# First MLP, first product: tiles 6 to 17 in pairs by seven block products instead of eight

## The reference

```python
h = x @ w_in                                   # first MLP: 2304x512 by 512x1024
e = np.exp(h - h_max)
sm = e / (np.sum(e, axis=-1, keepdims=True) + 1e-09)
solu = h * sm
ln = (solu - mu) / np.sqrt(var + 1e-06) * g_ln
x = ln @ w_out                                 # 1024x512
...
h = x @ w_in2                                  # second MLP: 512x2048
g = np.maximum(h, 0.0) + np.log1p(np.exp(-np.abs(h)))
out = g @ w_out2                               # 2048x512
```

## Time and profile before

| | us |
|---|---|
| median of 3 runs | 874.36 (874.33 to 874.37) |
| the profiled execution, its own time | 873.95 |
| its span, first to last instruction | 872.2 |
| first MLP's steady part, three tiles | 36.0 |
| TensorE busy | 859.9 (99% of the span) |
| VectorE, ScalarE, GpSimd busy | 633.8, 566.5, 345.2 |

### The profile page before, as it was taken

One profiled execution on the slowest core, in us unless ns is written; L12 is line 12 of the kernel. 1 busy time (PEld: TensorE's weight loads), 2 busy tenths in 40 slices (PEclk: granted clock), 3 DMA queues, 4 the chain that ended last, 5 costly groups with the idle time before them and its releaser, 6 DMA issues.

```text
span 872.2 us, 17032 instructions
## 1 busy us (share of the span) xinstructions
PE 859.9 (99%) x6357; PEld 721.1 (83%) x6357; DVE 633.8 (73%) x1215; ACT 566.5 (65%) x1040; POOL 345.2 (40%) x498
## 2 busy tenths in 40 slices
PE   7999999999999999999999999999999999999998
PEld 5666666666677989889899999999999999999997
DVE  7999999999937361543656778758768768858975
ACT  4888988888876352533464766667667666667664
POOL 4676888676626310201111322333323322333331
PEclk9999999999999999999999999999999999999999
DMA  6813441343002000000032300000100100000000
GB/s 170 221 49 83 90 111 34 85 104 126 2 2 61 13 1 1 1 1 1 1 97 83 136 1 20 18 0 2 37 1 2 37 1 1 36 0 0 36 0 36
DMA packets 30234, 37.03 MB, mean 42 GB/s; under 512 B 4688, under 2 KB 18384, under 8 KB 30160
## 3 DMA queue, kind: packets, MB, share of 16 engines
q1 hardware_dynamic: 29776, 35.89, 14.9%
q10 hardware_dynamic: 384, 0.16, 0.1%
HBM read 31.33 MB, written 4.72 MB: 41 GB/s over the span
## 4 chain that ended last, share of the span: by engine, by line
PE 90%; DVE 5%; issue 2%; ACT 1%; POOL 1%; DMA 0%; SPq 0%; DVEq 0%; ACTq 0%
PE m_ps L1181 23%; PE f_ps L1274 23%; PE h_ps L1065 12%; PE y_ps L1205 12%; PE s_ps L1097 8%; PE o_ps L1138 7%; DVE ntop L870 3%; PE t_ps L1113 2%; DVE kept L880 1%; PE lt_ps L1217 1%; PE s_ps L1092 1%; ACT expd L606 1%; POOL thresh L470 1%; POOL w_lo L454 1%; PE l_ps L1108 0%
## 5 line engine op out<-in xcount | busy, mean ns | idle before, releaser
L1181 PE MATMUL m_ps<-y_hi,w 128*128 128x384 f32 x768 | 211.8, 337 | 0.0
L546 POOL TENSOR_TENSOR w_lo<-w_rest,w_hi 128x512 fp32r<-128x512 f32 x82 | 107.1, 1306 | 247.3 <-ACT w_hi L729 247.3
L1181 PEld LDWEIGHTS m_ps<-y_hi,w 128*128 128x128 f32 x768 | 140.3, 188 | 3.9
L606 ACT ACTIVATE expd<-s_ps,ntop 128x576 f32<-128x576 f32 x144 | 105.7, 742 | 40.4 <-DVE ntop L870 39.4
L1181 PE MATMUL m_ps<-y_lo,w 128*128 128x384 f32 x384 | 129.0, 336 | 0.0
L729 ACT CAST w_hi<-w_rest 128x512 fp32r<-128x512 f32 x82 | 51.0, 622 | 107.2 <-PE f_ps L1274 102.8
L880 DVE SCALAR_TENSOR_TENSOR kept<-s_ps,thresh,expd 128x576 f32<-128x576 f32 x144 | 112.4, 817 | 3.7 <-POOL thresh L470 0.6
L870 DVE TENSOR_REDUCE ntop<-s_ps 128x1 f32<-128x576 f32 x144 | 106.8, 757 | 8.7 <-PE s_ps L1097 2.7
L1274 PE MATMUL f_ps<-w_hi,g_lo 128*128 128x512 f32 x282 | 111.5, 395 | 0.0
L1274 PE MATMUL f_ps<-w_hi,g_hi 128*128 128x512 f32 x282 | 110.8, 393 | 0.0
L1274 PE MATMUL f_ps<-w_lo,g_hi 128*128 128x512 f32 x282 | 110.4, 392 | 0.0
(11 more groups left out here) (96 smaller groups left out, 1695.2 us busy)
## 6 DMA issues: line engine op xcount, KB each, us to landing
q_sb<-q_t SPq DMA_DIRECT2D x28, 288.0 KB, 5.0
v_sb<-v_main SPq DMA_DIRECT2D x16, 256.0 KB, 3.2
stage<-w_in SPq DMA_DIRECT2D x16, 256.0 KB, 2.8
out<-o_sb SPq DMA_DIRECT2D x5, 768.0 KB, 3.6
w_rest<-w_out SPq DMA_DIRECT2D x7, 512.0 KB, 5.4
k_sb<-k_t SPq DMA_DIRECT2D x21, 144.0 KB, 4.7
stage<-w_in SPq DMA_DIRECT2D x4, 512.0 KB, 7.9
stage<-w_out SPq DMA_DIRECT2D x4, 512.0 KB, 6.7
```

The lines of the kernel that those rows point to most:

```text
L546: nc.gpsimd.tensor_tensor(w4[1][n % 2], w4_rows(n % F2, 1)[:, 0, :], f32(w4[0][n % 2]), ALU.subtract).then_inc(w4lo_made, 1)
L606: nc.scalar.activation(expd[:, tile % 2, :].rearrange("p (a b) -> p a b", a=2), s_ps[tile % 2][:, :, 0:HALF], ACT.Exp, bias=ntop[:, tile % ...
L1181: last = nc.tensor.matmul(m_ps[n % 4][:, 0:GC], w[n % F2][:, k, :], y[odd][:, k, :], start=(k == 0 and m == 0), stop=(k == C - 1 and m == 2))
```

## The change

Tiles 0 to 5 (`PLAIN`) stay as they are. Tiles 6 to 17 are taken in six pairs, p = 3 to 8: tiles a = 2p and b = 2p + 1. For a pair the first product is one of 2x2 blocks: the two tiles by the two halves of the inner dimension on one side, the two halves of the inner dimension by the two sides of `w1` on the other. It is made from seven block products of 6 matmuls of 128x512 each (2 blocks x 3), 42 in place of 48. For that:

- `w1` is loaded again, 4 pieces of 512 KB, into the four slots of `stage`; the second MLP's pieces are loaded after these are used up. VectorE makes four differences T1 to T4 (128x1024 each, L1221), ScalarE casts them (L957), GpSimd subtracts for the low parts (L666).
- For each pair GpSimd makes four sums S1 to S4 of 128x256 (L647); ScalarE casts those and the three plain blocks (seven casts of 128x256, L944 to L951) and VectorE makes seven low parts (L1229 to L1239). The four operands x_hi, x_lo, x_sum have one slot each, so they are made when the pair before has been multiplied.
- The seven products go to the four banks of `h_ps`; ScalarE copies three out (128x512, L963), VectorE makes four sums of a bank and a copy (L1252), GpSimd three sums of 128x512 (L653 to L658). The result lies in `solu`, in SBUF, and the row chain reads it there.
- The transpositions stand inside the pairs (`transposed_in`): pairs 3, 5, 6 and 8 have three each, pairs 4 and 7 none. The projection follows in two or four chunks.

The core of the diff:

```diff
             for n in range(C):
+                sp.wait_ge(w_lo, parts(C + n + 1))
+                sp.dma_start(staged(n)[0], staged_source(n)).then_inc(stage_in[n], 16)
+            sp.wait_ge(wsum_made, 4)
+            for n in range(W3, W_ITEMS):
...
+            def joins(p):
+                pool.wait_ge(summed, first(p, SUMS, 2))
+                pool.wait_ge(copied, first(p, COPIES, 2))
+                nc.gpsimd.tensor_tensor(p5_sb, w_sb, p5_sb, ALU.add).then_inc(joined, 1)
+                pool.wait_ge(copied, first(p, COPIES, 3))
+                nc.gpsimd.tensor_tensor(w_sb, w_sb, p7_sb, ALU.add).then_inc(joined, 1)
+                pool.wait_ge(joined, first(p, JOINS, 1))
+                pool.wait_ge(ln_made, 2 * p)
+                nc.gpsimd.tensor_tensor(solu[:, 1, half(1)], p5_sb, p7_sb, ALU.add).then_inc(joined, 1)
+
+            def w1_sum_low(n):
+                pool.wait_ge(wsum_hi, n + 1)
+                pool.wait_ge(wsum_made, (2, 3, 4, 4)[n])
+                hi, lo = (T1, T2, T4, T3)[n]
+                raw = (T1_raw, T2_raw, T4_raw, T3_raw)[n]
+                nc.gpsimd.tensor_tensor(lo, raw, f32(hi), ALU.subtract).then_inc(wsum_lo, 1)
+
+            for tile in range(PLAIN - 1):
+                norm(0, tile)
+            x_sums_of(PAIRED[0])
+            norm(0, PLAIN - 1)
+            for n in range(4):
+                w1_sum_low(n)
+            for p in PAIRED:
+                joins(p)
+                if p + 1 in PAIRED:
+                    x_sums_of(p + 1)
+                for tile in (2 * p, 2 * p + 1):
+                    norm(tile // 6, tile % 6)
...
+            def paired(p):
+                tiles = transposed_in(p)
+                if tiles:
+                    next_row(tiles[0])
+                if p == PAIRED[0]:
+                    pe.wait_ge(solu_made, PLAIN)
+                else:
+                    pe.wait_ge(copied, first(p - 1, COPIES, 3))
+                    pe.wait_ge(summed, first(p - 1, SUMS, 4))
+                pe.wait_ge(xp_lo, first(p, OPERANDS, 1))
+                product(0, A11, B11)
+                pe.wait_ge(xp_lo, first(p, OPERANDS, 2))
+                product(1, A12, B21)
+                pe.wait_ge(xp_lo, first(p, OPERANDS, 4))
+                pe.wait_ge(wsum_lo, 1)
+                product(2, S1, T1)
+                if tiles:
+                    next_row(tiles[1])
+                pe.wait_ge(xp_lo, first(p, OPERANDS, 5))
+                pe.wait_ge(wsum_lo, 2)
+                product(3, S2, T2)
+                pe.wait_ge(copied, first(p, COPIES, 1))
+                pe.wait_ge(xp_lo, first(p, OPERANDS, 7))
+                pe.wait_ge(wsum_lo, 4)
+                product(0, S3, T3)
+                pe.wait_ge(summed, first(p, SUMS, 1))
+                pe.wait_ge(xp_lo, first(p, OPERANDS, 6))
+                product(1, S4, B22)
+                if tiles:
+                    next_row(tiles[2])
+                pe.wait_ge(copied, first(p, COPIES, 2))
+                pe.wait_ge(wsum_lo, 3)
+                product(2, A22, T4)
...
+            for p in PAIRED:
+                paired(p)
+                if p % 3 == 0:
+                    project(2 * (p // 3) - 1, (0, 1))
+                elif p % 3 == 1:
+                    project(2 * (p // 3) - 1, (2, 3))
+                else:
+                    if p == PAIRED[-1]:
+                        next_row(MT - 3)
+                    project(2 * (p // 3), range(C))
```

More of the change, by code:

```diff
@@ L61 @@
 W4_LOADS = 4
+PLAIN = 6
+PAIRED = range(PLAIN // 2, TOKENS // (2 * P))
+COPIES, SUMS, JOINS, PRODUCTS, OPERANDS, STEPS = 3, 4, 3, 7, 7, 6
+PADDED = 16
 GR = 4
@@ L792, in _, with at, x_pair_high @@
                     w_high(C + n - 2)
[L793 to L797, removed]
+            def at(tile):
+                return tile // 6, tile % 6
+            def x_pair_high(p, n):
+                a, b = 2 * p, 2 * p + 1
+                if n == 0:
+                    if p == PAIRED[0]:
+                        act.wait_ge(h_made, PLAIN)
+                    else:
+                        act.wait_ge(products, first(p, PRODUCTS, 0))
+                    for part, k in ((A11, 0), (A12, 2)):
+                        nc.scalar.copy(part[0], x_rows(a, k)).then_inc(xp_hi, 1)
+                elif n == 1:
+                    nc.scalar.copy(A22[0], x_rows(b, 2)).then_inc(xp_hi, 1)
+                else:
+                    act.wait_ge(xsum_made, first(p, 4, n - 1))
+                    raw = (S1_raw, S2_raw, S4_raw, S3_raw)[n - 2]
+                    nc.scalar.copy((S1, S2, S4, S3)[n - 2][0], raw).then_inc(xp_hi, 1)
@@ new lines, in y_copy @@
+            def y_copy(group, m):
+                act.wait_ge(y_made, C * group + m + 1)
+                nc.scalar.copy(xt[:, group * C * GC + m * GC:group * C * GC + (m + 1) * GC],
+                               y_ps[m % 2][:, 0:GC]).then_inc(y_out, 1)
+            row_exponential(0, 4)
+            transposed_high(0, 2)
+            row_square(0, 4)
+            x_pair_high(PAIRED[0], 0)
+            x_pair_high(PAIRED[0], 1)
+            row_exponential(0, 5)
+            w1_sum_high(0)
+            for n in range(2, STEPS):
+                x_pair_high(PAIRED[0], n)
@@ new lines, in at, with w1_sum @@
+            def at(tile):
+                return tile // 6, tile % 6
+            def w1_sum(n):
+                if n == 0:
+                    for slot in range(C):
+                        dve.wait_ge(stage_in[slot], 48)
+                    dve.wait_ge(h_made, PLAIN)
+                if n in (1, 2):
+                    dve.wait_ge(wsum_made, n)
+                r11, r12, r21, r22 = w1_again
+                out, x, y = ((T1_raw, r12, r11), (T2_raw, r22, T1_raw), (T4_raw, r21, T2_raw), (T3_raw, r22, r12))[n]
+                nc.vector.tensor_tensor(out, x, y, ALU.subtract).then_inc(wsum_made, 1)
@@ new lines, in _ @@
+            for s in range(2, PLAIN):
+                tile = s - 2
+                dve.wait_ge(h_made, tile + 1)
+                row_top(tile, h_ps)
+                x_low(0, s)
+                row_solu(tile, h_ps)
+                if tile >= 2:
+                    transposed_low(0, tile - 2)
+            dve.wait_ge(h_made, PLAIN - 1)
+            row_top(PLAIN - 2, h_ps)
+            row_solu(PLAIN - 2, h_ps)
+            transposed_low(0, 2)
+            dve.wait_ge(h_made, PLAIN)
+            row_top(PLAIN - 1, h_ps)
@@ L1256, in _, with next_row, product @@
-            three_parts(pe, MT + 3, 6, mlp1, MT // 6 - 1)
+            def next_row(tile):
+                pe.wait_ge(ltlo_made, tile)
+                transpose_row(tile)
+            def product(bank, x, w):
+                for k in range(2):
+                    for n, (part, other) in enumerate(((0, 0), (0, 1), (1, 0))):
+                        last = nc.tensor.matmul(banks[bank], x[part][:, k, :], w[other][:, k, :],
+                                                start=(k == 0 and n == 0), stop=(k == 1 and n == 2))
+                last.then_inc(products, 1)
```

337 lines of the change are left out of this document (260 added, 77 removed).

## The result

The changed kernel takes **876.91 us** (median of 9 runs, 874.84 to 877.57) against 874.37 (874.15 to 875.57) for the kernel before on the same chip: ratio 1.0024, 95% interval 1.0014 to 1.0034. That is some 2 us slower, just beyond the 0.2% that a measurement can tell. The forecast was 875.5 within 872.6 to 879.0; by the prediction's own line of 876.1 the result counts as slower, to which it had given 0.44, against 0.48 for no difference. The profiled execution of the changed kernel took 877.52, its span 875.8 us, 3.6 more than the 872.2 of before.

What follows compares the result with a forecast made beforehand. TensorE, busy 99% of the span, was taken as the bound. From the profiled execution, 873.95 - 8.40 + 4.7 + 4.4 + 0.4 = 875.05; with 0.41 for the median, 875.5 us, range 872.6 to 879.0.

Steps and rivals of the forecast that it cites:

- What is removed: First MLP's first products: six pairs save 6 matmuls each, 36 x 0.233 = 8.40 us of TensorE time.
- Place 1: Pair 3: TensorE waits for GpSimd's low parts of T1 to T4, queued behind `ln` of tile 5; costs 4.7 us.
- The clock: TensorE in the first MLP: full granted clock expected, with nothing in the sum for a slower one.
- rival B: Pair 3, wait over 3 us: TensorE's clock halves, three products cost 4.2 us more; 879.7 us, chance 0.08.
- Place 2: Last transposition ahead of a projection, pairs 3, 5, 6, 8: TensorE waits for `ln_lo`; together 4.4 us.
- Place 3: First transposition in pairs 5 and 8: TensorE waits for the long row chain, 0.2 us each, 0.4 us.
- The second loading of w1: Loading w1 again in the first MLP: costed at nothing; up to 2 us if it lands 2 us later.
- Rival A: Row maxima reading `solu` in SBUF are held up by GpSimd's four sums: 3.0 us, 878.5 us, chance 0.13.
- C: Pair 3's low parts cost less and transpositions end 0.4 us earlier: 4.0 + 2.8 + 0 us, 872.8 us, chance 0.12.
- D: Whole change gives its full gain, as if no wait appeared: 866.0 us, chance 0.02.

Runs made afterwards that it cites:

- the doubled product: Kernel with GpSimd's low parts and the last transposition of a pair moved earlier, plus each pair's last product's six matmuls issued twice: 874.92 us.
- the version without waits: Changed kernel with GpSimd's low parts of T1 to T4 ahead of `norm` of tile 5 and a pair's last transposition one product earlier: 866.22 us.
- the wait filled: Changed kernel with ten more matmuls of 128x512 ahead of TensorE's wait for the low part of T3: 875.46 us.
- the two groups of runs behind 1.94: Changed kernel with only T1's low part ahead of GpSimd's `norm` of tile 5: 873.92 us; four runs 871.93 to 872.74, seven 873.75 to 874.35.
- the kernel with place 2 undone: Changed kernel with the last of a pair's three transpositions one product earlier and VectorE's low part ahead of the second total: 872.95 us.

## Why the prediction was right, and where not

- **What is removed**, 36 matmuls of 0.233 us, 8.40 us: right. 8.34 us by the doubled product, 8.50 by the version without waits.
- **Place 1**, 4.7 us in waits (ends 4.2 and 6.5; with nothing for the restart the prediction's own numbers give 4.4, not 4.2): right, 4.50. The chain came out link by link as told: `ln` behind the transposition, four low parts of 2.34 to 2.38 us, TensorE at its product 11.6 us behind the start of the transposition, where the prediction had 11.9.
- **The clock** behind place 1: the step that failed. The forecast had full clock, with a wait of over 3 us in it, and nothing in the sum for a slower one; a drop stood as rival B at 0.08, and among the signs of being wrong. It happened, at 1.56 us rather than B's 4.2, for nine matmuls rather than three products of 1.4 us more each. B's mechanism was right, its chance too small and its size too large. The Trainium skill, TensorE: Matmul & The Clock Gate, The HAM clock gate, says that inactivity lowers the clock. The runs agree: with the wait filled the granted clock stays at 1.00, and the stretch is 1.56 us shorter.
- **Place 2**, 4.4 us (ends 3.6 and 5.0): right in place and cause, 3.97 us. From the start of the transposition to the projection it took 3.08 us, where the prediction had 3.3; in the changed kernel, pair 3:

```profile
322.13 0.71 PE L1540 MATMUL lt_ps<-ident,ln 64*128 64x64 f32 x16
...
325.21 0.44 PE L1526 MATMUL y_ps<-ln_hi,w_hi 128*128 128x384 f32 x1 [0.77 <-DVE ln_lo L1162]
```

- **Place 3**, 0.4 us (ends 0 and 1.0 each): 0, but only just. TensorE needs the low part of the first transposed tile ahead of the second transposition, and there is no wait there in pairs 5 and 8. Pair 5 of the changed kernel, the low part and the second transposition:

```profile
355.51 1.22 DVE L1162 TENSOR_TENSOR ln_lo<-lt_ps,ln_hi 128x1024 fp32r<-128x1024 f32 x1 [2.59 <-ACT ln_hi L823]
...
356.87 0.71 PE L1540 MATMUL lt_ps<-ident,ln 64*128 64x64 f32 x16
```

  The low part ends 0.14 us before TensorE starts, 13.2 us behind the pair before, where the prediction had 13.4. That nearness is in part luck: the durations that it lists up to the end of `solu` of b add up to 10.1, not 9.6, which would have made the place 0.7 us each; the trace has 9.4, since neighbouring operations of VectorE overlap a little.
- **The second load**, nothing: right. The run with it alone shows that the transfers cost nothing; and in the changed kernel, where VectorE waits for them, TensorE has no wait between 280 us and pair 3.
- **The end**, +0.7 us: in no step. I had written that the second MLP is not touched and that what the first MLP gains or loses reaches the end unchanged. It does up to the last copy, 418.80 us in both; behind it the changed program takes longer.
- **Rival A**, the row maxima held up by GpSimd's sums: out. In the changed kernel VectorE's maximum at 325.67 us took 1.21 beside two of GpSimd's four sums, and so did the one of pair 8 at 435.16, beside which GpSimd does nothing. GpSimd there:

```profile
325.32 0.73 POOL L647 TENSOR_TENSOR x_sum_raw<-x_lo_raw,xt 128x256 f32<-128x256 f32 x1
326.14 0.74 POOL L647 TENSOR_TENSOR x_sum_raw<-xt,x_sum_raw 128x256 f32<-128x256 f32 x1
```

VectorE's maxima:

```profile
325.67 1.21 DVE L1182 TENSOR_REDUCE st<-solu 128x1 f32<-128x1024 f32 x1
...
435.16 1.21 DVE L1182 TENSOR_REDUCE st<-solu 128x1 f32<-128x1024 f32 x1
```

  The rule that the prediction named beside it (the Trainium skill, SBUF - State Buffer, Who interferes with whom: a `tensor_reduce` doesn't contend) is borne out by these rows.
- **Rivals C and D**: neither. Of C's terms, 4.0, 2.8 and 0, only the last came (4.50, 3.97 and 0 were measured); D is what the version with both edits reaches, 866.22 us for the 866.0 told.

The sum by the measured terms, for the stretch from tile 5 to W3, is -8.50 + 4.50 + 1.56 + 3.97 = +1.53 us, and +1.55 was read. That they agree is no test, since the four terms are differences between the same five profiles; the doubled product is the one check from outside, 8.34 for the 8.50. To it come 0.7 at the end, so +2.2 without the chance at the start; the medians say +2.5 and, the second time, +1.9. The forecast of +1.1 was too low by the clock and the end, some 2.3 us, and too high by 0.2, 0.4 and 0.4 at the three places. The misses partly cancelled, which is luck, so the forecast's distance of 1.4 us says less than the terms.

## What to carry to other kernels

A faster algorithm for one operation pays by its operands' way as much as by its count: here 8.4 us of saved matmuls were lost to four low parts that stood behind a wait they had no need of, and to a transposition one product too late, and two moves in the lists brought all of it back. Where TensorE is the bound and a change puts a wait of 2 to 3 us before it, count the slower clock behind it on top of the wait: here 1.56 us behind 3.02, and some 1.8 us between the two groups of runs behind 1.94. Where the wait is sure, the chance for it isn't small. And read the stretch behind the last computation in both profiles: it isn't the same for two programs merely because the last stage is.

## What the hardware showed that I had not expected

- TensorE fell to half its clock (steps of 0.43 us for 0.233) behind waits of 3.02 and 1.94 us, behind the latter in only some of the runs, and behind none of 0.81 and 0.90 us. It came back after nine slow steps in the changed kernel (3.73 us), after eight in the second profile of it, and later in the kernel with place 2 undone, where a transposition lay among the products. The changed kernel's runs spread over 2.7 us, and the clock is a part of that: the fastest, 874.84 us, had a mean clock of 0.999, all others 0.996 or 0.997. It isn't the whole, since 875.54 and 877.52 us both had 0.997.
- With ten matmuls put into the wait whose results nobody reads, the kernel was faster by 1.0 to 1.5 us.
- The stores of the last tiles took 2.7 us in place of 2.2, and the end of the program 0.7 us longer, with one fetch of code there and a tail of 0.75 us at the rate of one DMA engine. What puts the fetch there is open.
